# Attention and two gated layers on one core: a split value product, GpSimd normalisation, a straight-line order and a kv load into own buffers

## The reference

```python
kv_pool = kv.reshape(B, H // 4, 4, W // 4, 4, C).mean(axis=(2, 4))   # 768 keys
k = v = kv_pool.reshape(B, -1, C) @ w_sr
s = (q @ k.T) / sqrt(C);  s = s - s.max(-1)
a = exp(s);  a /= a.sum(-1) + 1e-9
x = a @ v                                                   # attention
h = x @ w_in1;  g = max(h, 0) + alpha * min(h, 0);  x = g @ w_out1
h = x @ w_in2                                               # d_ff = 2048
g = (a0 + a1 h + a2 h^2 + a3 h^3) / (1 + |b0||h| + |b1|h^2 + 1e-6)
out = g @ w_out2
```

## Time and profile before

| | |
|---|---|
| median of three runs | 1656.17 us (1656.15 to 1659.51) |
| profiled execution, its own time | 1657.08 us |
| its span, first to last instruction | 1655.3 us |
| first product of the scores / of the first layer | 54.34 us / 371.68 us |
| PE busy | 1573.5 us (95%) |
| DVE, ACT, POOL busy | 1415.9, 1371.3, 1075.3 us |

### The profile page before, as it was taken

The page is one execution under the profiler, slowest core; times in us unless marked ns, Lnnn a source line. Parts: engine busy times, 40 slices in busy tenths (PEclk is TensorE's granted clock), DMA queues, the critical chain, the costliest instruction groups (busy, mean ns, idle before and its releaser), DMA issues. The chain is left out here.

```text
span 1655.3 us, 21951 instructions
## 1 busy us (share of the span) xinstructions
PE 1573.5 (95%) x5615; PEld 976.7 (59%) x5615; DVE 1415.9 (86%) x2172; ACT 1371.3 (83%) x2611; POOL 1075.3 (65%) x1160
## 2 busy tenths in 40 slices
PE   2799999998999999999999999999999999999976
PEld 2577777764555655556555556555565556555543
DVE  5666767651999999999999999999999999999997
ACT  2455555542999999999999999999999999999996
POOL 0011111110888888888888888888888888888887
PEclk9899999999999999999999999999999999999998
DMA  8100000000000000000000000000000000000000
GB/s 231 57 23 22 19 19 19 19 0 0 1 7 7 1 7 7 7 7 1 7 7 7 7 1 7 7 7 7 1 7 8 7 7 1 7 7 7 7 7 7
DMA packets 12278, 24.27 MB, mean 15 GB/s; under 512 B 1536, under 2 KB 1680, under 8 KB 11920
## 3 DMA queue, kind: packets, MB, share of 16 engines
q1 hardware_dynamic: 10896, 19.93, 3.9%
q10 hardware_dynamic: 1280, 3.22, 0.6%
HBM read 16.85 MB, written 6.29 MB: 14 GB/s over the span
## 5 line engine op out<-in xcount | busy, mean ns | idle before, releaser
L260 POOL TENSOR_TENSOR area<-area 128x512 f32<-128x512 f32 x384 | 493.4, 1285 | 220.8 <-ACT area L400 174.6
L642 PE MATMUL banks<-x_hi,win_lo 128*128 128x512 f32 x768 | 508.6, 662 | 24.2 <-DVE area L574 15.5
L252 POOL TENSOR_TENSOR area<-area 128x512 f32<-128x512 f32 x288 | 369.1, 1282 | 35.6 <-PE banks L809 12.7
L800 PE MATMUL banks<-neg_part,wout 128*128 128x512 f32 x768 | 388.1, 593 | 0.2 <-ACT neg_part L378 0.2
L809 PE MATMUL banks<-area,wout 128*128 128x512 f32 x768 | 378.0, 600 | 4.1 <-POOL area L252 4.0
L560 DVE SCALAR_TENSOR_TENSOR banks<-area,abs_b,banks 128x512 f32<-128x512 f32 x384 | 282.2, 752 | 60.0 <-ACT banks L394 58.0
L644 PE MATMUL banks<-x_hi,win_hi 128*128 128x512 f32 x768 | 303.7, 395 | 0.0
L643 PE MATMUL banks<-x_lo,win_hi 128*128 128x512 f32 x768 | 303.2, 395 | 0.0
L574 DVE SCALAR_TENSOR_TENSOR area<-banks,ab_raw,area 128x512 f32<-128x512 f32 x384 | 285.1, 742 | 1.3 <-ACT area L414 1.2
L566 DVE SCALAR_TENSOR_TENSOR banks<-banks,ab_raw,area 128x512 f32<-128x512 f32 x384 | 279.7, 751 | 0.0
L400 ACT ACTIVATE area<-banks,ab_raw 128x512 f32<-128x512 f32 x384 | 267.9, 698 | 0.0
(11 more groups left out here) (77 smaller groups left out, 1704.6 us busy)
## 6 DMA issues: line engine op xcount, KB each, us to landing
area<-in_kv_dram SPq DMA_DIRECT2D x24, 256.0 KB, 5.7
area<-in_q_dram SPq DMA_DIRECT2D x24, 256.0 KB, 2.7
out_dram<-area SPq DMA_DIRECT2D x24, 256.0 KB, 2.0
area<-in_moe_w_in_dram ACTq DMA_DIRECT2D x2, 1024.0 KB, 11.8
neg_part<-in_w_sr_dram ACTq DMA_DIRECT2D x1, 64.0 KB, 12.3
al_rows<-in_moe_alpha_dram ACTq DMA_DIRECT2D x1, 8.0 KB, 5.4
ab_raw<-in_moe_a_dram ACTq DMA_DIRECT2D x1, 2.0 KB, 7.7
ab_raw<-in_moe_b_dram ACTq DMA_DIRECT2D x1, 1.0 KB, 9.3
```

The lines of the kernel that those rows point to most:

```text
L252: nc.gpsimd.tensor_tensor(rational[:, m % 3, :], newton[:, m % 2, :], ratio[:, m % 2, :], ALU.mult).then_inc(s["rat_done"], 1)
L260: nc.gpsimd.tensor_tensor(cubic[:, m % 2, :], sq[:, m % 2, :], lin_p[:, m % 2, :], ALU.mult).then_inc(s["cubic_done"], 1)
L642: nc.tensor.matmul(dst, w[1], x[0], start=start, stop=False)
L800: nc.tensor.matmul(banks[:, ACC1, :], wout1[:, c, :], neg_part[:, n % 2, :], start=False, stop=(c == BLOCKS - 1)).then_inc(s["m1_done"], 1)
```

## The change

Memory: the tiles of attention and of the layers become tensors of their own; a tensor `early` holds, during the load stage, all six kv chunks, the raw `w_in1`, its transpose, the pooled chunks and `w_sr`. `w_in2` is now fetched into `wout2`'s place and split after attention; `w_out2` follows it. `DVE_PIXELS` is 8: DVE adds eight pixels of a key, PE adds the other eight and DVE's sum by nine fp32 products with the identity, which also transpose. Keys and values are made chunk by chunk. Values are split. The order of a step is the same on all 26 steps, without a loop; queries are turned at the beginning of their own step.

```diff
 sync:
+  sp.dma_start(raw_in[0], w_in1)                     # was on ACT's queue
   for c in range(CHUNKS):
-    after(sp, s["pooled_done"], c - 1)
+    if c == 3: sp.dma_start(wout1[:], w_out1...)     # was on ACT's queue
     for r in range(4): sp.dma_start(kv_in[:, c, ...], kv_rows[...])   # was kv_in[:, c % 2, ...]
-  sp.wait_ge(s["lin_ready"], 1);  q groups 0 and 1   # now on ACT's queue, after w_sr, alpha, a, b
-  sp.wait_ge(s["v_done"], 2);  sp.dma_start(wout2[:], w_out2...)
+  sp.wait_ge(s["v_lo_done"], 2);  sp.dma_start(raw_in[1], w_in2)
   (loop over the other q groups)
+  sp.wait_ge(s["in2_lo_done"], 1);  sp.dma_start(wout2[:], w_out2...)

 gpsimd:
+  def normalise(g, t):
+      n, b = g * TILES + t, t % 2
+      pool.wait_ge(s["inv_done"], n + 1)
+      after(pool, s["pt_ready"], (g - 1) * CHUNKS)
+      nc.gpsimd.tensor_scalar(probs[:, g % 2, t, :], expd[:, b, :], inv_sum[:, b:b + 1], 1.0,
+                              ALU.mult, ALU.mult).then_inc(s["probs_done"], 1)
+  for g in range(STEPS):                             # GROUPS + 2
+      shift(g, 0); normalise(g - 1, 3); shift(g, 1); guard(g, 0); guard(g, 1); shift(g, 2)
+      normalise(g, 0); guard(g, 2); shift(g, 3); normalise(g, 1); normalise(g, 2); guard(g, 3)

 scalar, attention (exps(g, t) also waits for probs_done and eps_done of tile n - 2):
+  query_hi(g); probs_hi(g - 2, 2); probs_hi(g - 2, 3); exps(g - 1, 3); probs_hi(g - 2, 4)
+  exps(g, 0); probs_hi(g - 2, 5); exps(g, 1); probs_hi(g - 1, 0); attended_hi(g - 2)
+  probs_hi(g - 1, 1); exps(g, 2)
+  after the last step: weight_hi(raw_in[1], win2_hi, "in2")

 vector, load stage:
   def pool_keys(c):
-    nc.vector.tensor_reduce(pooled[:, c % 2, :], kv_in[:, c % 2, :] ... j=PIXELS)
+    nc.vector.tensor_reduce(pooled[:, c, :], kv_in[:, c, 0:DVE_PIXELS * P] ... j=DVE_PIXELS)
 vector, attention:
+  def probs_lo(g, c):
+      dve.wait_ge(s["pt_hi_done"], g * CHUNKS + c + 1)
+      nc.vector.tensor_tensor(pt_lo[:, c % 2, :], banks[:, P_T[c % 2], :], pt_hi[...], ALU.subtract)
+  query_lo(g); probs_lo(g - 2, 2); maxima(g, 0); probs_lo(g - 2, 3); inverse(g - 1, 3)
+  probs_lo(g - 2, 4); maxima(g, 1); probs_lo(g - 2, 5); inverse(g, 0); maxima(g, 2); inverse(g, 1)
+  probs_lo(g - 1, 0); attended_lo(g - 2); probs_lo(g - 1, 1); maxima(g, 3); inverse(g, 2)
+  at g == GROUPS: the scaling of wout1 (was in the load stage)
+  after the last step: weight_lo(raw_in[1], win2_hi, win2_lo, "in2")

 tensor, load stage:
   def pooled_transpose(c):
-    nc.tensor.transpose(banks[:, 4 + c % 2, 0:P], pooled[:, c % 2, :], ident[:])
+    for j in range(DVE_PIXELS, PIXELS):
+        nc.tensor.matmul(dst, kv_in[:, c, j * P:(j + 1) * P], ident[:], start=(j == DVE_PIXELS), stop=False)
+    nc.tensor.matmul(dst, pooled[:, c, :], ident[:], start=False, stop=True)
+  key_chunk(c): one key product; at c = 2 and c = 5 also three value products
+  turn_in1(); pooled_transpose(0); queries(0); pooled_transpose(1); key_chunk(0); pooled_transpose(2)
+  key_chunk(1); linear_weight(); then for c in 3, 4, 5: pooled_transpose(c), key_chunk(c - 1); key_chunk(5)
 tensor, attention:
   def weighted(g, c):
-    nc.tensor.matmul(banks[:, ATT, :], values[:, c, :], probs_t[:, c % 2, :], ...)
+    split_product(banks[:, ATT, :], (v_hi[:, c, :], v_lo[:, c, :]), (pt_hi[:, c % 2, :], pt_lo[:, c % 2, :]), ...)
+  queries(g); weighted(g - 2, 0); weighted(g - 2, 1); transposed(g - 2, 3); tile_scores(g, 0)
+  transposed(g - 2, 4); weighted(g - 2, 2); tile_scores(g, 1); weighted(g - 2, 3)
+  transposed(g - 2, 5); weighted(g - 2, 4); tile_scores(g, 2); transposed(g - 1, 0)
+  weighted(g - 2, 5); transposed(g - 1, 1); tile_scores(g, 3); transposed(g - 1, 2)
+  (weighted(g, c) waits for pt_lo of chunk c, transposed(g, c) for pt_lo of chunk c - 2)
```

More of the change, by code:

```diff
@@ L142, in build, with group @@
         block = ctx.enter_context(nc.Block())
[L144 to L155, removed]
+        def group(g):
+            return 0 <= g < GROUPS
+        STEPS = GROUPS + 2
         def real(m):
@@ L227, in attention, with shift @@
[L227 to L239, removed]
+            def shift(g, t):
+                if group(g):
+                    n, b = g * TILES + t, t % 2
+                    pool.wait_ge(s["max_done"], n + 1)
+                    after(pool, s["exp_done"], n - 1)
+                    nc.gpsimd.tensor_tensor(exp_shift[:, b:b + 1], neg_max[:, b:b + 1], scale_col[:],
+                                            ALU.mult).then_inc(s["shift_done"], 1)
@@ L241, in correction @@
+            for g in range(STEPS):
+                shift(g, 0)
+                normalise(g - 1, 3)
+                shift(g, 1)
+                guard(g, 0)
+                guard(g, 1)
+                shift(g, 2)
+                normalise(g, 0)
+                guard(g, 2)
+                shift(g, 3)
+                normalise(g, 1)
+                normalise(g, 2)
+                guard(g, 3)
             def correction(m):
@@ new lines, in in1_transposed, with weight_hi @@
+            def in1_transposed():
+                for n in range(4):
+                    act.wait_ge(s["in1_t_ready"], n + 1)
+                    nc.scalar.activation(w_in1_t[:, 4 * n:4 * n + 4, :].rearrange("p b c -> p (b c)"), banks[:, n % 2, :],
+                                         ACT.Copy).then_inc(s["in1_t_done"], 1)
+            def weight_hi(raw, hi, name):
+                act.wait_ge(s[f"ld_{name}"], 16)
+                nc.scalar.activation(hi[:], raw, ACT.Copy).then_inc(s[f"{name}_hi_done"], 1)
@@ new lines, in exps @@
+            def exps(g, t):
+                if group(g):
+                    n, b = g * TILES + t, t % 2
+                    act.wait_ge(s["s_ready"], n + 1)
+                    act.wait_ge(s["shift_done"], n + 1)
+                    after(act, s["probs_done"], n - 1)
+                    after(act, s["eps_done"], n - 1)
+                    nc.scalar.activation(expd[:, b, :].rearrange("p (h n) -> p h n", h=2), scores(b), ACT.Exp,
+                                         bias=exp_shift[:, b:b + 1], scale=SCALE,
+                                         accum_out=exp_sum[:, b:b + 1]).then_inc(s["exp_done"], 1)
@@ L300, in _ @@
+            in1_transposed()
             copy_pooled_t(0)
[L302 to L305, removed]
+            query_hi(0)
+            weight_hi(raw_in[0], win1_hi, "in1")
             copy_pooled_t(1)
-            act.wait_ge(s["ld_in2"], 16)
-            nc.scalar.activation(win2_hi[:], raw_in[1], ACT.Copy).then_inc(s["in2_hi_done"], 1)
+            act.wait_ge(s["lin_ready"], 1)
@@ L309, in _ @@
+            nc.scalar.activation(lin_hi[:], banks[:, 1, 0:P], ACT.Copy).then_inc(s["lin_hi_done"], 1)
             copy_pooled_t(2)
[L310 to L324, removed]
@@ new lines, in turn_in1, with linear_weight @@
+            def turn_in1():
+                pe.wait_ge(s["ld_in1"], 16)
+                for n in range(4):
+                    after(pe, s["in1_t_done"], n - 1)
+                    for j in range(4):
+                        c = 4 * n + j
+                        last = nc.tensor.transpose(banks[:, n % 2, j * P:(j + 1) * P], raw_in[0][:, c * P:(c + 1) * P], ident[:])
+                    last.then_inc(s["in1_t_ready"], 1)
+            def linear_weight():
+                pe.wait_ge(s["in1_t_done"], 4)
+                pe.wait_ge(s["ld_out1"], 16)
+                for c in range(BLOCKS):
+                    last = nc.tensor.matmul(banks[:, 1, 0:P], w_in1_t[:, c, :], wout1[:, c, :], start=(c == 0), stop=(c == BLOCKS - 1))
+                last.then_inc(s["lin_ready"], 1)
@@ new lines, in transposed @@
+            def transposed(g, c):
+                if group(g):
+                    if c == 0:
+                        pe.wait_ge(s["probs_done"], (g + 1) * TILES)
+                    after(pe, s["pt_lo_done"], g * CHUNKS + c - 1)
+                    for t in range(TILES):
+                        last = nc.tensor.transpose(banks[:, P_T[c % 2], t * P:(t + 1) * P],
+                                                   probs[:, g % 2, t, c * P:(c + 1) * P], ident[:])
+                    last.then_inc(s["pt_ready"], 1)
```

511 lines of the change are left out of this document (249 added, 262 removed).

## The result

The changed kernel takes 1617.4 us in the median (1616.42 to 1617.97, four runs), against 1656.58 for the kernel before in the same series. The ratio is 0.9758, 95% interval 0.9745 to 0.977. 1621 was predicted, in a range of 1610 to 1640. Its profiled execution took 1616.42 us, 40.7 less than that of before.

A forecast was written before the change was run, and what follows sets the result against it. PE bounds attention and the layers, a chain of transfers, pooling and products the load stage. Load 42.5 + attention 292.1 + layers 1283.6 + 1.4 between = 1619.6 us of span, plus 1.8: 1621 us, range 1610 to 1640.

The forecast's parts named there:

- Step of attention: One of attention's 26 repeated steps: 11.7 us predicted against 13.02 before, from 11.46 of PE work plus slip and misfits.
- T, S and W: PE's work in an attention step: four-tile turn 0.44 us, a tile's scores 1.06, value product 0.69 as three fp32r passes.
- the slip: 0.15 in front of S0: In each attention step, tile 0's scores on PE start about 0.15 us late, waiting for queries behind DVE's list.
- Even the dear price fits: POOL's normalisation in attention: 0.94 us expected, but even at 1.93 us each the step's order was said to have room.
- written-out step: Attention step laid out slot by slot across engines with hand-overs; only the queries' slot had under 0.5 us of room.
- Rival D: POOL bounds attention's steps; break-even at 3.0 us a normalisation, 1687 us in all at 3.3 us; chance 0.04.
- Ends of attention: Attention's first two and last two steps, without full PE load: 17.4 plus 17.3 us, 34.7 against 31.0 before.
- Load stage: First score of attention at 42.5 us against 54.34, -11.8; last chunk landing at 35, PE possibly later.
- Between the stages: Between attention and layers, w_in2's split on ACT delays the first layer's block 1 from 2.4 to about 3.8 us: +1.4.
- C: Rival: no slips, attention steps of 11.46 us and first score at 39 us, 1612 us in all; chance 0.13.
- A and E: Rivals on attention's steps: interlocking lists, 12.4 us a step, 1636 us, chance 0.15; late code fetch, 1632 us, chance 0.04.
- B: Rival: load stage gains little, transfers or PE's identity products hold it to 49 us, 1628 us in all; chance 0.11.

The follow-up runs named there:

- run 5: Changed kernel with the value product as one fp32 product again, low parts left out of it: 1643.67 us.
- run 2: Changed kernel with each POOL normalisation done twice: 1635.3 us, ratio to the kernel before 0.9867.
- run 4: Doubled POOL normalisations as in run 2, with tile 0's normalisation put in front of tile 2's shift in POOL's list: 1623.24 us.
- run 8: Changed kernel with one more 1 MB transfer (w_in2) in front of w_out1 and kv chunk 3: 1618.49 us, first score at 43.35 us.
- run 3: Changed kernel with each POOL normalisation done three times, load stage as changed: 1711.99 us.
- run 6: Changed kernel with DVE adding all 16 pixels of a key and PE only transposing the sum: 1623.49 us, first score at 43.99 us.
- runs 7 and 8: Changed kernel with each kv chunk's transfer waiting until PE pooled the chunk two before, 1622.46 us; and with an extra 1 MB transfer, 1618.49 us.

## Why the prediction was right, point by point

- **Step of attention.** Predicted 11.7, measured 11.48. The PE sum of 11.46 held to 0.02 us, with T, S and W as priced; run 5 confirms the split's 0.96. The mis-sized term is the slip: 0.15 in front of S0 and a remainder of 0.09, in all 22 x 0.22 = 4.8 us too much. I had summed DVE's list by durations (9.9 us). The starts show that a 0.69 us subtraction holds the list for 0.60 and a 0.95 us maximum for 0.87, as the next one starts before the record ends; by starts it is 4 x 0.87 + 4 x 0.18 + 8 x 0.60 = 9.0 us, and the windows give 9.3 a step (161.4 of 200 us). So the queries' low part starts 1.26 us behind the turn instead of 1.6, right behind ACT's high part, and S0 does not wait.
- **POOL.** The price 0.94 was right (0.91). "Even the dear price fits" was wrong: run 2 paid 0.57 us a step at 1.89 us. The written-out step had moved only guard(3), shift(0) and exponential(0) of the next step and let the rest stand. But exponential(2) stood 0.2 us behind normalise(0), which at the dear price ends 1 us later; run 2 shows exponential(2) waiting 1.05 us for it and exponential(3) 0.82 us for the next normalisation, and run 4, which only moves normalise(0) up by one place, takes most of it back. That the delay also feeds itself once round the loop is argued, not shown by itself. Rival D's break-even of 3.0 us is therefore mis-sized too: a straight line between 1.89 us (step 12.05) and three times, about 2.9 us (15.28), passes 13.3 us at about 2.3 us, which is an estimate from two points. So the rule of the Trainium skill that the prediction weighed ("GPSIMD Engine Reference", section 4.1) would matter more than I gave it where work has two inputs: at that price 18 us of the gain are lost (run 2), unless the list is reordered (run 4). The other half of that rule of the Trainium skill, that one-input work on GpSimd is roughly at line rate, is borne out by the trace only in part: POOL's normalisation is 0.91 us, and DVE's in the kernel before was 0.62:

```profile
L516 DVE TENSOR_SCALAR area<-area,inv_sum 128x768 f32<-128x768 f32 x74 | 46.0, 621 | 2.6
```

- **Ends of attention.** 34.7 predicted; 286.55 - 22 x 11.48 = 34.0. Step 25 stands behind the scaling as predicted.
- **Load stage.** 42.5 predicted, 42.46 met in this execution, 41.3 in the mean: near, but by luck: in this execution two errors cancel. A product with new weights is 3.81 / 16 = 0.24 us, not 0.33: the 0.33 of the earlier trace rows came behind 5.2 us of idle, and run 8 shows the same price (5.44 us for 16) with the clock at the half level for part of it. So PE is not late. The transfers were: they ran at 212 / 0.80 = 265 GB/s of busy time, not 285, and 8.98 MB / 265 + 3.7 = 37.6 us is about where the last chunk became usable (37.2), not 35. In run 3, with the faster transfers, PE began the last chunk at 35.12, as predicted, and the first score came at 40.37: the 2.1 us between that and 42.5 are PE's work priced too high.
- **Between the stages.** +1.4 predicted, 2.90 - 1.76 = +1.14 met. The 3.8 us from block 0 to block 1 were 3.13 (329.01 to 332.14), because the 2.4 of before included the record that begins early. The layers as a whole are +1.7; the other 0.6 is not traced to a place and is small beside their spread of 1284.5 to 1289.4.
- **Sum.** Against 1619.6 us of span, 1614.3: -5.5 in attention, +0.3 in the layers, nothing in the load stage. Of the rivals, the pure PE step of C (11.46) happened, its early first score (39) did not. A and E would show in the steps, and twenty of them lie within 0.02 us of each other; B's 49 us and D's full POOL (it is busy 87 of 200 us) did not come.

## What to carry to other kernels

Sum the bounding engine by start-to-start spacing, and the others too: summing their durations invents slips. A written-out step is a good proof that a list fits at one price, and a poor one at another: carry a delay once round the loop before calling it hidden. Work moved out of one stage should be given an idle stretch by name; two pieces moved to the end of attention cost 3.3 us by the medians (0.9 and 1.45 of it seen in the traces) that idle stretches elsewhere gave back.

## What the runs showed that was not expected

- The price of a matmul read behind an idle of some 5 us is up to 1.4 times that of a steady one (0.33 against 0.24 us), and in the kernel before the windows still showed a granted clock of 1.00 over that stretch, though only seven matmul records start in a microsecond there, as at the half level in run 8:

```profile
33.00:34.00 1.00, 1.00 (x7) 1.00 (x6) 1.00 (x1) 0.00 (x0) 0.00 (x0) 1.00 0.90 305
```

- At a tripled normalisation the step grew by 3.8 us while POOL was busy 79% of the time: an order, not an engine, was the bound.
- The first score moved by 2.1 us between executions of the same load stage, with transfers at 261 to 294 GB/s.
- Taking work off PE in the load stage (run 6) or making it wait (runs 7 and 8) cost twice: PE's next products ran at the half level, 1.2 GHz.
